# Exchanging the halves of a complex state by on-chip transfers instead of a product with a constant matrix

## What is computed

```python
a_re_n, a_im_n = (a_re * scale, a_im * scale)      # |a| at most 0.999
for t in range(S):
    ar, ai = (a_re_n[:, :, t, :, None], a_im_n[:, :, t, :, None])
    new_re = ar * S_re - ai * S_im
    new_im = ar * S_im + ai * S_re
    kv = np.einsum('bhd,bhe->bhde', k[:, :, t], v[:, :, t])
    S_re, S_im = (new_re + kv, new_im)
    y[:, :, t] = np.einsum('bhd,bhde->bhe', q[:, :, t], S_re)
```

## Time and profile before

| | |
|---|---|
| three timed runs | 752.48, 755.88, 760.36 us (median 755.88) |
| the profiled execution | 751.82 us, of which the span of the profile is 749.8 us |
| granted TensorE clock, mean over the span | 0.998 of full speed |
| TensorE matmul busy | 662.7 us (88%), 5226 instructions |
| VectorE busy | 614.0 us (82%), 1165 instructions |
| ScalarE busy | 410.4 us (55%), 747 instructions |
| recurrence of batch 1 | from about 258 to 291 us, of batch 2 from 426 to 459, of batch 3 from 593 to 627 |

### The profile page before, as it was taken

The page is one execution under the profiler, slowest core; times in us unless marked ns, Lnnn a source line. Parts: engine busy times, 40 slices in busy tenths (PEclk is TensorE's granted clock), DMA queues, the critical chain, the costliest instruction groups (busy, mean ns, idle before and its releaser), DMA issues.

```text
span 749.8 us, 13183 instructions
## 1 busy us (share of the span) xinstructions
PE 662.7 (88%) x5226; PEld 501.4 (67%) x5226; DVE 614.0 (82%) x1165; ACT 410.4 (55%) x747; POOL 0.2 (0%) x4
## 2 busy tenths in 40 slices
PE   0006989999999999999999999999999999999998
PEld 0002768776666788776566788776566888998765
DVE  3999998999999787998989787998988675773663
ACT  6404367434667656335668647335667335654565
POOL 0000000000000000000000000000000000000000
PEclk9999999999999999999999999999999999999999
DMA  8704785200049464100058464100055440000001
GB/s 342 270 0 119 203 244 189 93 0 1 0 121 271 121 181 159 61 0 1 0 142 258 124 175 167 48 1 0 1 147 170 131 128 2 1 0 1 2 22 43
DMA packets 93628, 73.84 MB, mean 98 GB/s; under 512 B 8704, under 2 KB 85760, under 8 KB 92928
## 3 DMA queue, kind: packets, MB, share of 16 engines
q1 hardware_dynamic: 93568, 73.01, 32.1%
HBM read 49.34 MB, written 23.65 MB: 97 GB/s over the span
## 4 chain that ended last, share of the span: by engine, by line
PE 53%; DVE 32%; ACT 7%; issue 3%; DMA 3%; SPq 0%; DVEq 0%; ACTq 0%
DVE cv L1138 6%; PE wide L1603 6%; PE wide L1448 5%; PE wide L1584 5%; PE bank L1655 4%; PE wide L1639 4%; PE bank L1663 4%; PE wide L1460 3%; PE wide L1513 3%; DVE m L956 3%; PE wide L1534 3%; DVE heads L1143 3%; PE wide L1579 2%; DVE m L955 2%; PE wide L1575 2%
## 5 line engine op out<-in xcount | busy, mean ns | idle before, releaser
L1513 PE MATMUL wide<-x_hi_lo,win_hi 128*128 128x384 f32 x384 | 107.7, 350 | 3.4 <-DVE x_hi_lo L1102 2.6
L1513 PEld LDWEIGHTS wide<-x_hi_lo,win_hi 128*128 128x128 f32 x384 | 69.8, 188 | 7.7 <-issue 4.6
L1534 PE MATMUL wide<-heads,wout 128*128 128x384 f32 x200 | 70.1, 494 | 4.8 <-DVE heads L1143 4.8
L1202 DVE TENSOR_REDUCE nmax<-wide 128x1 f32<-128x768 f32 (+2 forms) x96 | 55.3, 618 | 21.1 <-PE wide L1613 21.0
L1138 DVE SCALAR_TENSOR_TENSOR cv<-h,wconv,cv 128x768 f32<-128x768 f32 x64 | 64.9, 1014 | 9.0 <-ACT cv L681 7.4
L1603 PE MATMUL wide<-attn 64*128 64x512 f32 (+3 forms) x256 | 65.0, 482 | 2.3 <-ACT attn L705 2.3
L1513 PE MATMUL wide<-x_hi_lo,win_lo 128*128 128x384 f32 x192 | 64.5, 336 | 0.0
L729 ACT ACTIVATE xs<-wide 128x896 f32<-128x896 f32 x48 | 44.1, 918 | 37.1 <-PE wide L1639 37.1
L655 ACT ACTIVATE h<-wide 128x384 f32<-128x384 f32 x64 | 29.6, 490 | 56.0 <-PE wide L1513 29.2
L1422 PE MATMUL wide<-attn,ident 128*128 128x512 f32 x4 | 3.9, 1082 | 62.3 <-ACT m L620 62.3
L1534 PEld LDWEIGHTS wide<-heads,wout 128*128 128x128 f32 x200 | 36.6, 189 | 30.5 <-DVE heads L1143 10.3
(11 more groups left out here) (205 smaller groups left out, 1505.1 us busy)
## 6 DMA issues: line engine op xcount, KB each, us to landing
heads<-heads_dram SPq DMA_DIRECT2D x96, 192.0 KB, 3.6
araw<-a_in SPq DMA_DIRECT2D x12, 768.0 KB, 6.2
araw<-qk_in SPq DMA_DIRECT2D x12, 768.0 KB, 4.7
heads_dram<-m SPq DMA_DIRECT2D x18, 384.0 KB, 3.6
heads_dram<-araw SPq DMA_DIRECT2D x18, 384.0 KB, 2.9
v<-v_in SPq DMA_DIRECT2D x4, 1536.0 KB, 6.7
out_dram<-h SPq DMA_DIRECT2D x24, 192.0 KB, 2.1
heads_dram<-m SPq DMA_DIRECT2D x12, 192.0 KB, 2.8
```

Source lines behind the costliest of these rows:

```text
L1202: dve.tensor_reduce(nmax[:, t, side:side + 1], slot_scores(t, side), AXX, ALU.max, negate=True).then_inc(s_nm, 1)
L1513: last = MM(low[u % 2][:, 0:NT], w[:, k, mt * P:(mt + 1) * P], xs[:, k, n * NT:(n + 1) * NT], start=(k == 0 and part == 0), stop=(k == KT ...
L1534: last = MM(mlp_bank[u][:, 0:NT], wout[:, mt, k * P:(k + 1) * P], hgate(mt)[:, n * NT:(n + 1) * NT], start=(mt == 0), stop=(mt == MT - 1))
```

## The change

From batch 1 on, TensorE no longer makes J U. SyncE waits for `uu` and issues two transfers from SBUF to SBUF, each of 48 partitions x 384 columns (73.7 KB), which write the halves of `uu` into `turned` in exchanged places. VectorE reads `turned` instead of PSUM, multiplies it with a column of signs and im(g) in one instruction, and the last addition becomes a subtraction. The signs are made once, in batch 0, by a sum over the columns of `rot`. Batch 0 works as before. The load of the exponential table in batches 1 and 2 moves from behind `copy_k` of chunk 1 to the start of `main(b)`. The wait for ScalarE's copy of the last results, which `rotate` did for the bank b7, moves to the first product of the feed-forward block.

```diff
+            def turn_state(b, c):
+                sp.wait_ge(s_u, GAINS * b + c + 1)
+                for part in range(2):
+                    sp.dma_start(turned[part * D:(part + 1) * D, :],
+                                 uu[(1 - part) * D:(2 - part) * D, :]).then_inc(s_tu, 16)
...
             def main(b):
                 more = b + 1 < B
+                if b:
+                    turn_state(b, 1)
                 load_heads(b, 3)
                 if b:
                     outputs_stored(b - 1)
+                    turn_state(b, 2)
                 else:
                     store_first_chunk(2)
                     load_a(1, 1)
                 load_heads(b, 4)
-                if b == 0:
+                if b:
+                    turn_state(b, 3)
+                else:
                     store_unit(0, 2)
                 load_heads(b, 5)
-                if b == 0:
+                if b:
+                    turn_state(b, 4)
+                else:
                     load_a(1, 2)
...
                     store_unit(b + 1, UNITS - 1)
+                    turn_state(b + 1, 0)
                 if b + 2 < B:
                     load_a(b + 2, UNITS - 1)
...
+                if b and more:
+                    exp_tables()
                 for c in range(NC):
                     if c + 1 < GAINS:
                         copy_k(b, c + 1)
                     if b and more and c < UNITS - 1:
-                        if c == 0:
-                            exp_tables()
                         ln(b + 1, c)
                         guess(b + 1, c)
...
                 TT(by_head(g1), by_head(uu), col(0), ALU.mult).then_inc(s_g1, 1)
-                dve.wait_ge(s_j, n + 1)
                 new = st[:, (c + 1) % 2, :, 0:D]
-                TT(new, by_head(b7[0:2 * D, 0:DM]), col(1), ALU.mult).then_inc(s_g1, 1)
+                if b == 0:
+                    dve.wait_ge(s_j, n + 1)
+                    TT(new, by_head(b7[0:2 * D, 0:DM]), col(1), ALU.mult).then_inc(s_g1, 1)
+                else:
+                    dve.wait_ge(s_si, 1)
+                    dve.wait_ge(s_tu, 32 * (n - GAINS + 1))
+                    STT(new, by_head(turned), sign[:], col(1), ALU.mult, ALU.mult).then_inc(s_g1, 1)
                 dve.wait_ge(s_g1, 2 * n + 2)
-                TT(new, new, by_head(g1), ALU.add).then_inc(s_st, 1)
+                TT(new, by_head(g1), new, ALU.add if b == 0 else ALU.subtract).then_inc(s_st, 1)
...
                             norm_step(1, 1, 0)
+                            dve.wait_ge(s_const, 80)
+                            dve.tensor_reduce(sign[:], rot[:], AXX, ALU.add).then_inc(s_si, 1)
...
+                if mt == 0:
+                    pe.wait_ge(s_fe[1], PAIRS * b + 1)
...
-                    if c + 1 < NC:
+                    if b == 0 and c + 1 < NC:
                         rotate(b, c)
```

More of the change, by code:

```diff
@@ L110, in program @@
         eps = sb("eps", [P, 1])
+        sign = sb("sign", [2 * D, 1])
         win_hi = sb("win_hi", [P, KT, FF], F32R)
@@ L169, in program @@
         assert o <= E * S
+        turned = attn[0:2 * D, o:o + DM]
         win_staged = [attn[:, o:o + FF], h[:].rearrange("p b s -> p (b s)")[:, 0:FF], stage[:]]
@@ L292, in program @@
         s_j = sem("state_rotated")
+        s_tu = sem("state_halves_turned")
+        s_si = sem("sign_of_halves")
         s_g1 = sem("state_parts")
```

## The result

The change made the kernel slower: 770.28 us, median of five runs (769.62 to 778.13), against 755.88 us, median of five of the kernel before (751.74 to 761.46). The ratio is 1.0205, with an interval of 1.0149 to 1.026. A second measurement of the same kernel gave 1.0245 (1.0202 to 1.0288). I had forecast 752.3 us in a range of 747 to 758.

A forecast was written before the change was run, and what follows sets the result against it. In the recurrence a chunk's chain was taken to run through TensorE alone. Removed rotations 3.93 us, less stalls 1.07 and 0.75 and signs 0.2, gave 1.9 us off 754.2: 752.3 us, range 747 to 758.

The forecast's parts named there:

- The gain from the product: Recurrence, batches 1 to 3: removing the rotation wins 0.20 us in chunk 0, 0.37 in chunks 1 to 3; 3.9 us in all.
- The period: Time per chunk of the recurrence in batches 1 to 3: falls from 6.81 to 6.44 us.
- the hand-over: From ScalarE's copy of transposed k to TensorE's gain: taken as 0.15 us, between bounds of 0.06 and 0.35.
- Scores of chunk 3 wait for their loads in batches 1 and 2: Chunk 1's pair delays chunk 3's loads by 0.5 us; TensorE stalls 1.07 and 0.75 us, none in batch 3.
- The transfers' own time: SBUF to SBUF, issue to landing: 2.1 us; turned halves 2.7 us after U, inside 4.35 us, so no cost.
- The rival in which this ring is the bound: Chunks 0 to 3 of each batch: U, transfer and three VectorE steps close a 7.65 us ring; 764 us, chance 0.09.
- The new step: VectorE's instruction reading `turned`: 0.55 us like the one it replaces, 0.05 either way, under cover of slack.
- The stall priced at its own length: TensorE ahead of chunk 3's scores: idle 1.07 and 0.75 us in batches 1 and 2, subtracted as such in the sum.
- The rest: Table load hidden, gate steps and output copy cost and gain 0, moved wait already fulfilled; only the signs cost 0.2 us.
- the signs: Batch 0: the sum making them is one VectorE instruction of 96 x 96, 0.2 us (0 to 0.55).
- The table load: Start of `main`: ScalarE's 1.28 us load hides in 1.62 us of idle time ahead of its copy, 0.3 us to spare.
- loads of chunk 3 later than 0.5 us behind their old place: SyncE's loads ahead of chunk 3's scores: starting over 0.5 us late was named as showing the forecast wrong.

The follow-up runs named there:

- e7: Changed kernel without transfers and without the exchange of halves, signs tile declared behind the large tiles: 752.82 us, ratio 0.998 to the kernel before.
- e14: Changed kernel with the signs in their old place but in a slot of 256 bytes per partition: 759.17 us, ratio 1.0049 to the kernel before.
- e10: Changed kernel, signs declared last, chunk 1's pair of transfers issued behind the loads of chunk 3: 774.27 us, ratio 1.0286 to the kernel before.
- e1: The changed kernel again, unaltered, for a second profile: 772.84 us, ratio 1.0245 to the kernel before.
- e5: Kernel before plus one unused tile behind eps, moving all tiles behind it by 32 bytes: 766.28 us, ratio 1.0148.
- e6: Changed kernel, whole, with the signs tile declared behind the large tiles: 764.36 us (752.15 to 766.3), ratio 1.0037 from four shorter runs.
- e9: Kernel before with the transfers made and waited for beside TensorE's rotation, whose result is used; signs declared last: 757.32 us, ratio 1.0049.
- e13: Kernel before with an unused tile of 128 bytes per partition behind eps, all tiles behind it 128 bytes higher: 759.85 us, ratio 1.0061.
- e11: Changed kernel, no tile shifted, GpSimd's queue issuing the pairs instead of SyncE's: 762.82 us, ratio 1.012 to the kernel before.
- e12: Kernel before with only `heads`, the tile of loaded q and k, 32 bytes off: 762.78 us, ratio 1.0119.
- e2: Changed kernel with chunk 1's pair of transfers issued behind the loads of chunk 3: 785.89 us, ratio 1.038 to the kernel before.

## Why the prediction was wrong

- **The gain from the product: right.** The period was forecast at 6.44 us and is 6.41 in `e7`; the hand-over was taken as 0.15 us and is 0.14; batch 3 wins 1.1 us for the 1.3 forecast.
- **Scores of chunk 3 wait for their loads in batches 1 and 2: right in kind, too small.** I had 1.07, 0.75 and 0 us for batches 1 to 3. Measured were 2.39, 1.78 and 1.34 us after, and 1.58, 1.41 and 0.53 us in `e14`, where the tiles are in place. Against the start of the scores of chunk 2, my sum has the loads 0.9 us late (264.4 against 263.72 - 0.20 = 263.52); they start 1.15 us late, since each issue of the pair takes 0.59 us, not 0.47. Then they land in up to 6.0 us instead of 5.1. Even without any pair, the stalls in `e7` are 0.83 and 1.27 us, where my numbers give 0.57 and 0.25: I had taken the landing times of the earlier trace rows as fixed.
- **The transfers' own time: nearly right.** 2.4 us to landing in the median for 2.1, and VectorE never waits for them after (in `e14` three times, 3.5 us in all). The rival in which this ring is the bound does not describe the kernel; it does describe `e10`. The new step takes 0.61 us, not 0.55, under cover.
- **The stall priced at its own length: wrong.** The sum had 1.07 us for 1.07 us of idle time. A stall of 2.39 us was followed by 12 us at 0.57 of the clock. The forecast had no term for that, and by it small delays of loads can become microseconds. They do not always: the stall of 1.34 us in batch 3 had full clock behind it, and so did the two in `e1` and `e14` that were longer (1.73 and 1.58 us).
- **"The rest": the step that failed.** It priced the signs as one VectorE instruction, 0.2 us. The instruction is lost in the scatter; the tile that it writes costs about 12 us (766.28 against 754.33 in `e5`, and 1.48% of the 2.05%). I had put the move of all tiles behind it, which the full diff shows in its first line, at nothing. `e14` says what the change does without it: 759.17 us, 0.5% slower, where I had said 0.3% faster. So the sum over queue, stalls and gain was itself some 6 us too low (by `e6`, up to 12), of which `e9` shows 3.4 as the price of the transfers.
- **The table load: right.** ScalarE's table load lies in its idle time, from 269.55 to 270.83, and the copy behind it starts only at 271.16, released by the transposes.

The profile's signs for "wrong" that I had named include this one: loads of chunk 3 later than 0.5 us behind their old place.

A page bears on it that I had not weighed. The Trainium skill, page "DMA: Bandwidth & Descriptors", section "How a descriptor splits into AXI transactions", says that pieces of 256 bytes start at multiples of 256, and that a descriptor that starts elsewhere costs extra beats. By that rule a run of 512 bytes, 32 bytes off, touches three such blocks instead of two. The page words it for what is read; here the shifted tile is written by the loads. The runs agree in kind (offset 0 and 256: 3.6 us, offset 32: 4.3 us). The rule alone would have 128 bytes cost as many blocks as 32, and by an estimate with the page's beats of 32 bytes even more than 32 (20 beats against 17, with 16 in place). `e13` is cheaper (4.1 us, 0.6%): the measurement decides.

**What stays open.** How the loss that is left in `e14` and `e6` divides between SyncE's queue and the traffic; `e11` shows that it is not the queue alone. Why an offset of 128 bytes costs less than one of 32. Why `e6`, which differs from `e14` only in where `sign` lies, gave a median 5 us higher. Its longer runs had a mean clock of 0.98, its shorter ones 0.987 to 0.995, and the profiles show one of each kind: in `e6` (764.63 us) the scores of chunk 3 wait 2.08 and 2.63 us in batches 1 and 2, the clock falls behind both, and the recurrences take 38.2 and 36.2 us; in `e14` (756.52 us) they wait 1.58 and 1.41 us at full clock, and the recurrences take 33.8 and 33.6 us. What makes a run one or the other stays open. So does the place of the pairs' own tiles: `uu` and `turned` begin off a multiple of 256 bytes in every kernel here, and none was run with them on one. The effect of the clock was seen in each profile and not taken away by itself.

## What to carry to other kernels

A tile added in the middle moves all tiles behind it: before reading a diff as so many instructions, look at the addresses of the tiles that transfers write and read, and declare small tiles behind the large ones, or in slots of 256 bytes. Where a load lands just as it is wanted, with no slack, a delay is not priced at its own length, since the clock can fall behind the stall. And moving work off TensorE onto transfers pays only as far as the next waiter lets it: here 0.40 us (6.81 - 6.41) of 0.65 for each chunk, less than the transfers cost the loads.

## What the runs showed of the hardware

- **Where a tile starts in SBUF.** Transfers of 192 KB in runs of 512 bytes landed in 3.6 us with the tile at a multiple of 256 bytes, in 4.3 to 4.4 us at 32 bytes off, in 4.1 us at 128 off (kernels without the transfers). A packet of 512 bytes took 29.5, 35.6 and 33.5 ns in the mean. The whole kernel: 1.5% and 0.6%. Stores of 384 KB from `araw` slow down with the loads even where their own tile stays (3.9 us in `e12`); across the kernels they took 2.7 to 3.4 us with `heads` in place and 3.6 to 5.1 us with it off.
- **The clock behind a stall.** After idle times of TensorE of 1.78 us (`e5`), 2.39 us (after) and 2.95 us (`e10`) the granted clock was at the lower level for some 7, 10 and 12 us (11 x 0.31 / 0.5 in the stretch of `e5`, 12 x 0.43 / 0.5 after). That is no scale to price a stall by: behind 1.78 us in batch 2 after, the lower level lasted over 12 us (14 x 0.44 / 0.5), behind 2.98 us in batch 3 of `e10` some 3 us, and behind 1.73 us in `e1` and 2.51 us in `e11` the clock stayed at its upper level. The stretch of `e10` behind its stall:

```profile
282.00:294.00 12.00, 11.36 (x104) 10.18 (x104) 8.53 (x17) 0.98 (x2) 0.00 (x0) 0.50 0.33 86
```

- **Small transfers from SBUF to SBUF.** 72 KB land in 2.2 to 2.4 us from SyncE's queue in the median (2.7 and 2.8 us in `e10` and `e2`, where one pair of a batch stands behind loads) and in 3.2 us from GpSimd's, and issuing one took 0.59 us where a load of q and k takes 0.47.
